# Attention scores as plain fp32 matmuls, two heads on the two partition halves

## The reference

```python
scores = scale * np.matmul(q, k.transpose(0, 1, 3, 2))      # 4 batches x 8 heads, 576 x 576, depth 64
thresh = np.max(scores, axis=-1, keepdims=True) - tau
scores = np.where(scores >= thresh, scores, -1000000000.0)
scores = scores - np.max(scores, axis=-1, keepdims=True)
attn = np.exp(scores)
attn = attn / (np.sum(attn, axis=-1, keepdims=True) + 1e-09)
x = np.matmul(attn, v)                                       # then heads side by side: 2304 x 512
x = (s * np.maximum(x @ w_in, 0) ** 2 + b) @ w_out           # 512 -> 2048 -> 512
h = x @ w_in2
out = (h * (1.0 / (1.0 + np.exp(-1.702 * h)))) @ w_out2
```

## Time and profile before

| | us |
|---|---|
| median of 3 runs | 1175.69 (1175.53 to 1176.93) |
| profiled execution, first to last instruction | 1173.3 |
| PE busy | 1116.0 (95%) |
| DVE busy | 642.9 (55%) |
| ACT busy | 519.1 (44%) |
| POOL busy | 305.5 (26%) |

### The profile page before, as it was taken

The page is one execution under the profiler, slowest core; times in us unless marked ns, Lnnn a source line. Parts: engine busy times, 40 slices in busy tenths (PEclk is TensorE's granted clock), DMA queues, the critical chain, the costliest instruction groups (busy, mean ns, idle before and its releaser), DMA issues.

```text
span 1173.3 us, 18874 instructions
## 1 busy us (share of the span) xinstructions
PE 1116.0 (95%) x6688; PEld 1001.0 (85%) x6688; DVE 642.9 (55%) x1136; ACT 519.1 (44%) x1135; POOL 305.5 (26%) x324
## 2 busy tenths in 40 slices
PE   4799999999998999999999999899999999999998
PEld 3566666665668899999999999799999999999998
DVE  7998898989847763434434357742323233232322
ACT  3888888887863332322223233342323223232322
POOL 3867676777634400000000004420000000000000
PEclk9999999999999999999999999999999999999999
DMA  2323222222132310000000003310000000000000
GB/s 81 92 62 80 70 80 70 80 70 75 37 101 90 108 37 1 0 0 0 0 0 0 0 0 107 108 37 1 27 0 27 0 0 27 0 27 0 27 0 27
DMA packets 37931, 45.45 MB, mean 39 GB/s; under 512 B 22544, under 2 KB 25616, under 8 KB 37904
## 3 DMA queue, kind: packets, MB, share of 16 engines
q1 hardware_dynamic: 37904, 45.11, 12.6%
HBM read 40.37 MB, written 4.72 MB: 38 GB/s over the span
## 4 chain that ended last, share of the span: by engine, by line
PE 76%; DVE 11%; issue 6%; ACT 6%; SPq 0%; DMA 0%; ACTq 0%; POOL 0%; DVEq 0%
PE h_ps L271 31%; PE y_ps L372 30%; PE scores L290 6%; PE context L316 5%; DVE g_full L495 4%; PE turned L343 4%; DVE prob L430 3%; DVE neg_max L422 2%; ACT w_hi L540 2%; ACT limit L601 1%; DVE g_full L498 1%; ACT prob L596 1%; ACT gate L643 1%; DVE k_hi L464 1%; SPq L210 0%
## 5 line engine op out<-in xcount | busy, mean ns | idle before, releaser
L372 PE MATMUL y_ps<-g_hi,w_hi 128*128 128x384 f32 x768 | 258.0, 336 | 8.0 <-DVE g_lo L506 8.0
L271 PE MATMUL h_ps<-x_hi,w_hi 128*128 128x384 f32 x768 | 258.4, 336 | 6.6 <-POOL w_lo L744 5.5
L372 PE MATMUL y_ps<-g_hi,w_lo 128*128 128x384 f32 x768 | 257.3, 335 | 0.0
L372 PE MATMUL y_ps<-g_lo,w_hi 128*128 128x384 f32 x768 | 257.3, 335 | 0.0
L271 PE MATMUL h_ps<-x_hi,w_lo 128*128 128x384 f32 x768 | 256.7, 334 | 0.0
L271 PE MATMUL h_ps<-x_lo,w_hi 128*128 128x384 f32 x768 | 256.6, 334 | 0.0
L652 ACT CAST g_hi<-g_full 128x384 fp32r<-128x384 f32 x192 | 98.6, 514 | 332.7 <-PE y_ps L372 231.2
L506 DVE TENSOR_TENSOR g_lo<-g_full,g_hi 128x384 fp32r<-128x384 f32 x192 | 107.4, 559 | 224.7 <-ACT g_hi L652 224.7
L744 POOL TENSOR_TENSOR w_lo<-raw_slab,w_hi 128x1024 fp32r<-128x1024 f32 x29 | 69.2, 2388 | 367.4 <-ACT w_hi L540 367.4
L495 DVE TENSOR_TENSOR g_full<-gate 128x384 f32<-128x384 f32 x96 | 102.4, 1067 | 109.8 <-ACT gate L643 109.8
L271 PEld LDWEIGHTS h_ps<-x_hi,w_hi 128*128 128x128 f32 x768 | 144.1, 188 | 12.1 <-POOL w_lo L744 9.7
(11 more groups left out here) (46 smaller groups left out, 1111.8 us busy)
## 6 DMA issues: line engine op xcount, KB each, us to landing
q_raw<-q_t SPq DMA_DIRECT2D x64, 144.0 KB, 2.7
k_raw<-k_t SPq DMA_DIRECT2D x64, 144.0 KB, 2.8
raw_slab<-slabs_a SPq DMA_DIRECT2D x16, 512.0 KB, 3.2
raw_slab<-slabs_b SPq DMA_DIRECT2D x16, 512.0 KB, 3.2
out_t<-act SPq DMA_DIRECT2D x6, 768.0 KB, 3.5
v_sb<-v SPq DMA_DIRECT2D x32, 96.0 KB, 2.2
v_sb<-v SPq DMA_DIRECT2D x32, 48.0 KB, 2.2
consts<-tau SPq DMA_DIRECT2D x1, 0.5 KB, 2.3
```

The source lines that it names most:

```text
L271: mm = nc.tensor.matmul(bank[:, 0:TOK], wp[f][:, w], xp[:, c, :], start=(c == 0 and n == 0), stop=(c == DC - 1 and n == 2))
L372: mm = nc.tensor.matmul(y_ps[c][:, 0:TOK], wp[f][:, w], gp[:, f % 2, :], start=(f == 0 and n == 0), stop=(f == SLABS - 1 and n == 2))
```

## The change

The rounded copies are gone. `q_t` and `k_t` now hold pairs of heads: one head on partitions 0 to 63 and the other on 64 to 127, in one load each. Scores are plain fp32 matmuls on `q_raw` and `k_raw`, with the 64 partitions of one head each: side 0 into `scores[0]`, side 1 into `scores[1]`. So steps i and i+1 are now the same row block of the two heads of a pair, where they were two blocks of one head. DVE scales q once for a pair. The order of the four matmuls of a double step is new, and so is the place of the two waits for `masked`.

```diff
-LEAD_K_HI, LEAD_Q_SCALE, LEAD_Q_HI, LEAD_K_LO, LEAD_Q_LO = 8, 10, 6, 6, 4
+LEAD_Q_SCALE = 6
...
+def pair_at(i, lead):
+
+    return (i + lead) // PAIR_STEPS if (i + lead) % PAIR_STEPS == 0 else None
...
         def rows_of(j):
 
-            return CUTS[j % TPH], CUTS[j % TPH + 1] - CUTS[j % TPH]
+            t = j % PAIR_STEPS // 2
+            return CUTS[t], CUTS[t + 1] - CUTS[t]
...
+                        if not first:
+
+                            sp.wait_ge(scores_ready, STEPS * (it - 1) + PAIR_STEPS * (slot + 1))
+                        pair = 2 * it + slot
+                        sp.dma_start(q_raw[:, slot, :], q_t[pair]).then_inc(q_loaded[slot], 16)
+                        sp.dma_start(k_raw[:, slot, :], k_t[pair]).then_inc(k_loaded[slot], 16)
...
-                    if j % TPH == 0:
-
-                        pe.wait_ge(k_lo_ready, HEADS_PER_STEPS * it + slot + 1)
-                        pe.wait_ge(q_lo_ready, HEADS_PER_STEPS * it + slot + 1)
-                    if not (first and j < 2):
-
-                        pe.wait_ge(masked, base + j - 1)
-                    for n, k_part in enumerate((k_hi[slot], k_lo[slot])):
-                        for half in range(2):
-                            mm = nc.tensor.matmul(scores[j % 2][0:m, half, 0:HALF],
-                                                  q_hl[slot][:, q0:q0 + m],
-                                                  k_part[:, half * HALF:(half + 1) * HALF],
-                                                  start=(n == 0), stop=(n == 1))
-                    mm.then_inc(scores_ready, 1)
+                    if i % PAIR_STEPS == 0:
+
+                        pe.wait_ge(k_loaded[slot], 16 * (it + 1))
+                        pe.wait_ge(q_scaled, 2 * it + slot + 1)
+                    for half in range(2):
+                        for side in range(2):
+                            if half == 0 and not (first and i < 2):
+
+                                pe.wait_ge(masked, base + i + side - 1)
+                            d = slice(HEAD_DIM * side, HEAD_DIM * (side + 1))
+                            mm = nc.tensor.matmul(scores[side][0:m, half, 0:HALF],
+                                                  q_raw[d, slot, q0:q0 + m],
+                                                  k_raw[d, slot, half * HALF:(half + 1) * HALF],
+                                                  start=True, stop=True)
+                            if half == 1:
+                                mm.then_inc(scores_ready, 1)
...
-                        nc.vector.tensor_copy(k_hi[hr % HEADS_PER_STEPS][:], k_raw[:, hr % 2, :]
-                                              ).then_inc(k_hi_ready, 1)
...
-                        nc.scalar.copy(q_cut[hr % 2][64:128, :].bitcast(F32R), q_raw[64:128, hr % 2, :]
-                                       ).then_inc(q_hi_ready, 1)
...
-                        nc.gpsimd.tensor_tensor(k_lo[hr % HEADS_PER_STEPS][:], k_raw[:, hr % 2, :],
-                                                k_hi[hr % HEADS_PER_STEPS][:].bitcast(F32), ALU.subtract
-                                                ).then_inc(k_lo_ready, 1)
...
-                        nc.gpsimd.tensor_tensor(q_hl[hr % HEADS_PER_STEPS][:], q_raw[:, hr % 2, :],
-                                                q_cut[hr % 2][:], ALU.subtract).then_inc(q_lo_ready, 1)
```

More of the change, by code:

```diff
@@ L68, in steps_of, with group_at @@
 def steps_of(first, last):
-    return range(-max(LEAD_K_HI, LEAD_Q_SCALE) if first else 0, STEPS + (DRAIN if last else 0), 2)
-def head_at(i, lead):
+    return range(-LEAD_Q_SCALE if first else 0, STEPS + (DRAIN if last else 0), 2)
+def group_at(i, lead):
     return next((t // TPH for t in (i + lead, i + lead + 1) if t % TPH == 0), None)
+def pair_at(i, lead):
+    return (i + lead) // PAIR_STEPS if (i + lead) % PAIR_STEPS == 0 else None
 def build(nc, q_t, k_t, v, tau, slabs_a, slabs_b, s, b, out_t):
@@ L95, in build @@
         k_raw = sbuf(attn, "k_raw", [P, 2, SEQ])
[L96 to L99, removed]
         v_sb = sbuf(attn, "v_sb", [P, HEADS_PER_STEPS, TPH, HEAD_DIM])
@@ L199, in load_heads @@
             def load_heads(it, first, last):
-                for hr in range(HEADS_PER_STEPS + (HEADS_PER_STEPS if last else 0)):
-                    head = HEADS_PER_STEPS * it + hr
-                    slot = hr % 2
+                for hr in range(0, HEADS_PER_STEPS + (HEADS_PER_STEPS if last else 0), 2):
+                    slot = hr // 2 % 2
                     if in_range(hr, first, last, HEADS_PER_STEPS):
[L204 to L208, removed]
-                            for half in range(2):
-                                sp.dma_start(dst[64 * half:64 * half + 64, slot, :], src[head]
-                                             ).then_inc(loaded[slot], 16)
+                        if not first:
[3 more added lines that the diff above has]
+                        sp.dma_start(k_raw[:, slot, :], k_t[pair]).then_inc(k_loaded[slot], 16)
                         if first and hr == 0:
@@ L216, in load_heads @@
                     pair = hr // 2 - 2
-                    if hr % 2 == 0 and in_range(pair, first, last, 2):
+                    if in_range(pair, first, last, 2):
                         if not isinstance(it, int) or it > 1:
@@ L439, in attention @@
                         row_max(i + 1)
[L441 to L444, removed]
+                    pr = pair_at(i, LEAD_Q_SCALE)
+                    if pr is not None and in_range(pr, first, last, 2):
+                        dve.wait_ge(q_loaded[pr % 2], 16 * (it + pr // 2 + 1))
+                        nc.vector.tensor_scalar(q_raw[:, pr % 2, :], q_raw[:, pr % 2, :], -SCALE, None,
                                                 ALU.mult).then_inc(q_scaled, 1)
-                    hr = head_at(i, -TPH - 1)
+                    hr = group_at(i, -TPH - 1)
                     if hr is not None and in_range(hr, first, last, HEADS_PER_STEPS):
@@ L553, in store_turned @@
                         act_eng.wait_ge(context_ready, 4 * it + 2 * (pair - 1))
-                    nc.scalar.copy(prob_t[:, (j // TPH) % HEADS_PER_STEPS, 0:TPH - 1, q0:q0 + m],
+                    nc.scalar.copy(prob_t[:, head_of(j), 0:TPH - 1, q0:q0 + m],
                                    turned[:, 2 * (j % 2), 0:(TPH - 1) * m
@@ L563, in store_tails @@
                     act_eng.wait_ge(tail_ready, base + j + 2)
[L564 to L573, removed]
+                    q0, m = rows_of(j)
+                    h = head_of(j)
+                    nc.scalar.copy(prob_t[:, h:h + 2, TPH - 1, q0:q0 + m],
+                                   turned[:, 1, 0:2 * m].rearrange("p (h m) -> p h m", h=2)
+                                   ).then_inc(tail_stored, 2)
                 def store_context(u):
@@ L612, in attention @@
                     store_tails(i - LAG_TURN)
-                    hr = head_at(i, LEAD_Q_HI)
-                    if hr is not None and in_range(hr, first, last, HEADS_PER_STEPS):
-                        act_eng.wait_ge(q_scaled, HEADS_PER_STEPS * it + hr + 1)
-                        nc.scalar.copy(q_cut[hr % 2][64:128, :].bitcast(F32R), q_raw[64:128, hr % 2, :]
-                                       ).then_inc(q_hi_ready, 1)
                     if last and i == STEPS:
```

29 lines of the change are left out of this document (6 added, 23 removed).

## The result

The changed kernel takes 1199.61 us (median of 4 runs, 1197.35 to 1200.74) against 1175.61 (4 runs, 1174.85 to 1176.93). The ratio is 1.0202, 95% interval 1.0187 to 1.0216: it is slower by some 24 us, and 1200 was forecast.

What follows compares the result with a forecast made beforehand. Attention was taken to be bound by a loop through PE, DVE and ACT over two score buffers, 4.00 us a double step. Terms +24.9, +4.2 and -4.9 gave +24.2 on 1175.7, so 1200 us, range 1187 to 1225.

Steps and rivals of the forecast that it cites:

- What it moves: Attention's score loop: side 0's half 1 queues behind the second mask's wait, making a double step 4.29 us instead of 4.00.
- What it adds on PE: Scores on PE: fp32 row halves overlap, a full set takes 1.18 us, PE's work 3.7 us a double step, hardly changed.
- What it removes: k casts and half the q scalings on DVE, 42 us busy, plus POOL and ACT work; a gain only if DVE sets the pace.
- The scaling of q: On DVE between maxima and mask: delays the mask by 0.2 us once in five double steps.
- 75 double steps: Attention from step 8 to step 158: 299.9 us before, 324.8 after, +24.9.
- The first four: First four double steps, PE at the 1.2 GHz level: 5.1 us each, 20.4 against 16.2 before, +4.2.
- The start: Time to the first row maximum: 6.9 us instead of 11.76, -4.9, with scores 1.4 after k arrives.
- The drain: Work behind step 158, without scores: turns, contexts and norms keep their order, 0.
- the late record: Rival: side 0's half 1 starts one record late in each double step, 0.24 us more, 1219 us; chance 0.12.
- the missing overlap: Rival: row halves of the scores don't overlap on PE, 0.49 us more a double step, 1239 us; chance 0.10.
- The low clock: Rival: PE's pauses of 0.6 us a double step keep its clock low, time beyond 1380 us; chance 0.02.
- the first rival: The wait does not hold back side 0: 3.95 us a double step, about 1171 us; chance 0.08, 0.04 for no change.

Runs made afterwards that it cites:

- e2: The kernel before, rounded copies and fp32r matmuls kept, with only its score matmuls put in the change's half-by-half order: 1214.33 us, ratio 1.0315.
- e4: The changed kernel with the mask on exponents against exp(-tau), no limit operation, and PE waiting for the exponent instead of the mask: 1145.38 us, ratio 0.9739.
- e3: The changed kernel plus 31 DVE casts on spare tensors where the k_hi casts stood: 1200.10 us, ratio 1.0203.
- e9: The changed kernel plus POOL's two subtractions for each head, on spare tensors, where k_lo and q_hl stood: 1199.86 us, ratio 1.0199.
- e1: The changed kernel with both halves of side 0 ahead of the wait and of side 1's halves: 1190.15 us, ratio 1.0121.
- e7: e4 plus POOL's two subtractions for each head put back on spare tensors: 1194.53 us, ratio 1.0156.
- e8: e4 plus both the DVE casts and the POOL subtractions put back on spare tensors: 1206.45 us, ratio 1.0250.
- e5: The kernel before, rounded copies kept, with the same edit as e4: 1205.95 us, ratio 1.0257.

## Why the prediction was right

The mechanism was right: the second mask's wait ahead of half 1 of side 0 makes the loop longer. That 1199.6 was met to half a microsecond is luck in part, since errors of some 3 us cancel. Step by step, with the measured value of each term.

- **What it moves** was the deciding term and held: the wait for the second mask stands ahead of half 1 of side 0. Forecast 4.29 us a double step, measured 4.21 to 4.24 in three of five, 4.24 to 4.33 in the fourth and 4.55 in the fifth, 21.5 for ten steps against 21.6. e2 shows the order by itself to be a loss of 38 us.
- **What it adds on PE**: the row halves overlap, as the column halves of the earlier trace rows do; a set of scores is 1.24 us in e4 against 1.18 forecast. The Trainium skill (TensorE: Matmul & The Clock Gate, Part 3, "The mechanism") has small matmuls in different row groups run at the same time, and the trace agrees: in the changed kernel six records end 1.24 us after their load, where a row of six would take 1.72.
- **What it removes**: booked at nothing. For what fits the gap of 0.9 us that holds: e3 and e9 measure each part at nothing. "Its lighter load buys nothing" was too strong all the same. Behind the new order a long cast no longer fits: e2 has 4.94 us where it lies and the changed kernel 4.21. The sum is not touched, since its 4.29 has no cast in it. DVE's share was forecast at some 80% and is 73%.
- **The scaling of q** was charged 0.2 in ten steps, wrongly. In the rows above the mask follows the maximum by 216.62 - 214.87 = 1.75, as in a double step without scaling. The 0.2 in the earlier trace rows was ACT's q_cut ahead of the exponent, which is gone. Something else fills the place: once in ten steps ACT's copy of the context (L559) stands between the two exponents, the second mask waits 0.29 us for its limit, and that double step takes 4.55.
- **75 double steps**: forecast 324.8, measured 325.6 (26.62 to 352.17). Some 3.5 of that are a spell at the low clock level, below, which I had not in the sum; without it, as in e3 and e9 (322 in both), it is 2.7 less than forecast.
- **The first four**: forecast 20.4, measured 19.8 (6.84 to 26.62).
- **The start**: forecast 6.9 for the first maximum, measured 6.84, with two errors that cancel. k was there a microsecond earlier, since one load replaced two: scores start at 4.55. But in the first double step nothing of side 0 has run ahead, and the maximum comes 2.29 us after the load and not 1.4.

```profile
4.55 2.29 PE L289 MATMUL scores<-k_raw,q_raw 64*128 64x288 f32 x8 [4.55 <-DMA k_raw<-k_t]
```

- **The drain**: forecast 0. From the last maxima to the end are 1198.8 - 352.2 = 846.6 us, before 1173.3 - 327.8 = 845.5. That is 1 us more.

Of the rivals, the late record and the missing overlap would show maxima 4.5 and 4.8 apart throughout, and they are at 4.2. That the wait doesn't hold side 0 back is refuted by the load at 214.06 with its wait for DVE. The low clock is seen in one spell of attention only, below; contexts take 0.71 for a set of four behind it. The price that I had worked out for the first rival, 3.95 a double step, was too low all the same: e1 takes the hold away and gets 4.2 on average (20.85 for ten steps), because side 1, the contexts and turns and the next side 0 still stand behind the second mask. I had left PE's part of the loop out of that rival's sum. And the range leaves out 0.24 by my own chances, not 0.20: the 0.04 for no change lies outside it too.

By the Trainium skill (TensorE: Matmul & The Clock Gate, Part 3, "What overlaps and what doesn't"), as cited against that rival, matmuls start and end in program order. e1's trace differs. In its double step at 177.64, half 0 of side 1 is loaded and starts at 177.97, 0.05 after the second mask's end at 177.92; half 1 of side 0, which stands ahead of it in the program, starts at 178.23. What the changed kernel shows is narrower: none of the six records behind the second wait is loaded before 214.06, although the one ahead of them started at 213.54 and streams for 0.24.

## What to carry to other kernels

Before booking an engine's lighter load as gain, follow the loop over the buffers and see which instruction frees them and what stands ahead of the first one that needs them; interleaving two tiles to use the array better also ties each to the other's wait. A saving may be worth nothing in one order and 50 us in another: with the loop open, the work that the change takes off POOL is what makes e4 faster than the kernel before. And an engine that reads 97% busy may be waiting, or working at half its width, within a line of its records.

## What the runs showed of the hardware that I had not expected

**DVE and POOL hold each other up.** With one input of the mask in PSUM, masks take 816 ns and norms 820 (the changed kernel). With both in SBUF masks take 869 and norms 1253, up to 1.98 us for one (e4), and single masks reach 2.17 us (e7). A cast on DVE lasts 1.7 us instead of 0.45 beside a subtraction of POOL (the kernel before and e2). The Trainium skill (SBUF — State Buffer, "Who interferes with whom") says that a DVE instruction with two SBUF inputs contends with a GpSimd instruction that reads SBUF, which e4 to e8 agree with. The ranges for e4 and e5 left it out.

**A spell at the low clock.** The windows view of the changed kernel:

```profile
35.90:53.00 17.10, 16.39 (x62) 10.34 (x60) 11.40 (x24) 10.09 (x25) 5.15 (x8) 0.50 0.07 18
53.10:80.00 26.90, 26.31 (x167) 14.12 (x165) 18.92 (x41) 18.38 (x45) 10.26 (x18) 1.00 0.20 56
```

From 35.9 to 53.0 us the granted clock is 0.50, the 1.2 GHz level. Ahead of it PE did scores and turns of the first steps, without contexts, with pauses for the masks. It is not in every run: the profiled execution of e3 has no such spell in attention and reaches its last maxima at 348.78 instead of 352.17, so it is worth some 3.5 us. That is likely a part of the spread of the changed kernel's runs, 1197 to 1201.
